# Attention's running state made compact and updated in one step, and work reordered around the two joints of a three-stage kernel

## What is computed

```
for b in range(nb):                                   # attention, 2 batches, 8 heads, 768 tokens, 64 per head
    intra = einsum(qb, kb) * Dmask; intra = einsum(intra, vb)
    inter = einsum('bhid,bhde->bhie', qb * lam_pow, kv_state)
    out[:, :, sl] = intra + inter
    kv_state = lam_block * kv_state + einsum('bhsd,bhse->bhde', kb * rev_pow, vb)
x = out.transpose(0, 2, 1, 3).reshape(1536, 512)
for e in range(4):                                    # mixture of 4 experts, 512 -> 1024 -> 512
    out += p[:, e:e + 1] * (maximum(x @ w1[e], 0) @ w2[e])
a = x @ w1; b = x @ w2                                # gated product, 512 -> 1024
return (((a * b) @ w3) @ w_out)                       # w3 @ w_out is folded into one matrix first
```

## Times and profile before

| | us |
|---|---|
| median of 3 runs (796.08 to 797.36) | 796.5 |
| the profiled execution, its own time | 793.99 |
| its span, first to last instruction | 792.2 |
| PE busy in the span | 776.9 |
| DVE, POOL, ACT busy | 442.4, 439.7, 207.8 |

### The profile page before, as it was taken

How to read it: one execution, slowest core, us unless ns; L and a number is a source line. 1 busy time by engine, 2 the same in 40 slices (tenths; PEclk the granted TensorE clock), 3 DMA queues, 4 the chain that set the end, 5 groups by cost and what they waited for, 6 DMA issues and landing times.

```text
span 792.2 us, 9983 instructions
## 1 busy us (share of the span) xinstructions
PE 776.9 (98%) x3854; PEld 642.5 (81%) x3854; DVE 442.4 (56%) x627; ACT 207.8 (26%) x292; POOL 439.7 (56%) x389
## 2 busy tenths in 40 slices
PE   9999889999999999999999999999998899999998
PEld 7878768888888888888888888888886788888887
DVE  7549874554545545545545455456378653636356
ACT  7423331122222212221222122122234331223110
POOL 8837586557546565665575565656657533342500
PEclk9999999999999999999999999999999999999999
DMA  9977111010210110210100111101000200100004
GB/s 336 342 260 235 61 73 53 2 53 27 67 53 1 54 55 0 86 40 22 53 23 32 53 41 54 54 0 54 27 26 1 72 11 25 54 28 0 1 1 159
DMA packets 26590, 51.29 MB, mean 65 GB/s; under 512 B 3112, under 2 KB 9008, under 8 KB 26544
## 3 DMA queue, kind: packets, MB, share of 16 engines
q1 hardware_dynamic: 26384, 50.64, 18.9%
q10 hardware_dynamic: 160, 0.02, 0.0%
HBM read 45.38 MB, written 5.28 MB: 64 GB/s over the span
## 4 chain that ended last, share of the span: by engine, by line
PE 92%; DVE 4%; POOL 2%; issue 1%; ACT 0%; ACTq 0%; DVEq 0%
PE banks L1303 41%; PE banks L1276 27%; PE banks L1286 15%; PE banks L1189 5%; PE banks L1201 1%; DVE probs L869 1%; PE banks L1233 1%; PE banks L1225 1%; DVE qs L879 1%; POOL xs_l L524 1%; POOL hl L524 1%; PE banks L1249 0%; DVE t L908 0%; PE banks L1241 0%; POOL w_l L524 0%
## 5 line engine op out<-in xcount | busy, mean ns | idle before, releaser
L1010 DVE TENSOR_TENSOR acc<-banks,acc 128x512 f32<-128x512 f32 x215 | 147.1, 690 | 148.3 <-PE banks L1303 135.8
L524 POOL TENSOR_TENSOR hl<-ring,hh 128x512 fp32r<-128x512 f32 x96 | 138.3, 1454 | 162.1 <-ACT hh L630 162.1
L630 ACT ACTIVATE hh<-ring 128x512 fp32r<-128x512 f32 x120 | 75.7, 632 | 404.6 <-DVE ring L987 345.8
L524 POOL TENSOR_TENSOR w_l<-up_raw,w_h 128x1024 fp32r<-128x1024 f32 x43 | 103.4, 2406 | 90.8 <-ACT w_h L630 90.8
L1303 PE MATMUL banks<-hh,d_h 128*128 128x512 f32 x384 | 149.5, 389 | 2.0 <-POOL hl L524 2.0
L1303 PE MATMUL banks<-hh,d_l 128*128 128x512 f32 x384 | 149.4, 389 | 0.0
L1303 PE MATMUL banks<-hl,d_h 128*128 128x512 f32 x384 | 149.4, 389 | 0.0
L1276 PE MATMUL banks<-xs_h,w_h 128*128 128x512 f32 x336 | 131.2, 390 | 5.5 <-DVE u L968 4.7
L1276 PE MATMUL banks<-xs_h,w_l 128*128 128x512 f32 x336 | 130.8, 389 | 0.0
L1276 PE MATMUL banks<-xs_l,w_h 128*128 128x512 f32 x336 | 130.7, 389 | 0.0
L1303 PEld LDWEIGHTS banks<-hh,d_h 128*128 128x128 f32 x384 | 72.1, 188 | 17.3 <-issue 2.4
(11 more groups left out here) (139 smaller groups left out, 992.7 us busy)
## 6 DMA issues: line engine op xcount, KB each, us to landing
dn_raw<-in_moe_w SPq DMA_DIRECT2D x16, 512.0 KB, 3.3
up_raw<-in_moe_w SPq DMA_DIRECT2D x14, 512.0 KB, 3.3
w_raw<-in_w3T SPq DMA_DIRECT2D x16, 256.0 KB, 6.4
up_raw<-in_w SPq DMA_DIRECT2D x8, 512.0 KB, 3.3
pb<-route_scratch SPq DMA_DIRECT2D x12, 256.0 KB, 3.3
out<-acc SPq DMA_DIRECT2D x11, 256.0 KB, 2.0
wo_raw<-in_w_out SPq DMA_DIRECT2D x8, 256.0 KB, 5.3
chunk_w<-in_kT SPq DMA_DIRECT2D x8, 256.0 KB, 5.3
```

The lines of the kernel that those rows point to most:

```text
L524: return tt(dst, whole, high.bitcast(F32), ALU.subtract)
L630: return nc.scalar.activation(dst, src, ACT.Copy)
L1010: tt(cols, group_bank(g), cols, ALU.add).then_inc(acc_done, 1)
```

## The change

**State.** `state` becomes [128, HP, 64]: head 2p in rows 0 to 63 and head 2p+1 in rows 64 to 127 of column block p. `s_dec`, its POOL instruction, the semaphore `state_decayed` with its waits on DVE and SP, and the memset of `state` on POOL with its wait on DVE go. `keep_state` is one copy of 128x256 in a batch's first chunk, and otherwise four instructions that multiply by the decay and add the new part. `from_state` issues eight matmuls with 64 rows and 64 columns of the array each, where four took all of it. The two row halves of the array both write the one bank `out_bank(i)`, into different partitions.

**First joint and first runs.** The low part of `T2` is made half by POOL (k = 0) and half by DVE (k = 1, new semaphore `t2_lo`). POOL makes the third hidden low part of run 0 before `d_low(0)`, not after. In run 1 PE does P1 and P6 ahead of groups 0 to 3 of run 0, not between them; DVE takes `sum_u2(1)` ahead of those groups' evacuations.

**Second joint.** The sums for run NQ+1 move from DVE to POOL, right behind `a_low(NQ + 1)`; ACT's `s_high(NQ + 1)` moves from behind factor "P2" to between the copies of `B11` and `B21`; DVE's `weight_sums_low(NQ + 1)` moves from behind `sum_c22` to ahead of `t3_low(1)`.

```diff
-        state = place(c_at, "state", [P, HP, 2, D])
+        state = place(c_at, "state", [P, HP, D])
...
-                if 1 <= n < NT - 1:
-                    pool.wait_ge(state_ready, updates(i - 1))
-                    tt(s_dec..., state..., q_pow[:, :, P - 1:P].to_broadcast([P, HP, 2 * D]), ALU.mult)
...
-            t_low(0, T2, T2_AT)
+            pool.wait_ge(t_hi, 2)
+            low(xs_l[:, T2, 0, :], T2_AT[:, 0, :], xs_h[:, T2, 0, :]).then_inc(tp_lo, 1)
...
                 hidden_low(OUTS * w + 1)
-                d_low(w)
-                for k in range(2, OUTS):
+                if w > 0:
+                    d_low(w)
+                hidden_low(OUTS * w + 2)
+                if w == 0:
+                    d_low(w)
+                for k in range(3, OUTS):
                     hidden_low(OUTS * w + k)
...
             a_low(NQ + 1)
+            sums(NQ + 1)
...
             b_high(B11, slice(0, KH), slice(0, CW), grouped(NQ - 1, 0) - KH)
+            s_high(NQ + 1)
             b_high(B21, slice(KH, KT), slice(0, CW), grouped(NQ - 1, 0))
...
+                new = kv_bank[:, 0:HP * D].rearrange("p (a e) -> p a e", a=HP)
+                if n == 0:
+                    nc.vector.tensor_copy(state[:, :, :], new).then_inc(state_ready, 1)
+                    return
+                for a in range(HP):
+                    last = nc.vector.scalar_tensor_tensor(out=state[:, a, :], in0=state[:, a, :],
+                                                          scalar=q_pow[:, a, P - 1:P], in1=new[:, a, :],
+                                                          op0=ALU.mult, op1=ALU.add)
...
+            dve.wait_ge(t_hi, 2)
+            sub(xs_l[:, T2, 1, :], acc[:, 1, 0:CW], xs_h[:, T2, 1, :]).then_inc(t2_lo, 1)
...
+            weight_sums_low(NQ + 1)
             t3_low(1)
...
                         b22_low()
-                        weight_sums(w + 1)
...
-                for p in range(HP):
-                    last = mm(out_bank(i)[:, p * P:(p + 1) * P], state[:, p, :, :], qs[:, i % 2, p, :],
+                for h in range(H):
+                    p, r = divmod(h, 2)
+                    rows = slice(r * D, (r + 1) * D)
+                    last = mm(out_bank(i)[rows, p * P:(p + 1) * P], state[rows, p, :], qs[rows, i % 2, p, :],
                               start=False, stop=True, skip_group_check=True)
...
+                if w == 1:
+                    p1(w)
+                    p6(w)
+                    groups(w - 1, (0, 1, 2, 3))
```

More of the change, by code:

```diff
@@ L165, in attention_moe_projection @@
         probs = place(c_at, "probs", [P, H, P])
-        s_dec = place(c_at, "s_dec", [P, HP, 2, D])
         decay = place(c_at, "decay", [P, H, P])
@@ L241, in attention_moe_projection @@
         blank_ready = sem("blank_ready")
-        zeros_ready, state_zero, pow_ready, route_ready = (
-            sem("zeros_ready"), sem("state_zero"), sem("pow_ready"), sem("route_ready"))
+        zeros_ready, pow_ready, route_ready = sem("zeros_ready"), sem("pow_ready"), sem("route_ready")
         pool_chain, dve_chain = sem("pool_chain"), sem("dve_chain")
@@ L477, in _ @@
             nc.gpsimd.memset(zeros[:, :], 0.0).then_inc(zeros_ready, 1)
-            nc.gpsimd.memset(state[:, :, :, :], 0.0).then_inc(state_zero, 1)
             A = stack[:, 0, :]
@@ L535, in _ @@
                        ALU.mult).then_inc(k_decayed, 1)
-                if 1 <= n < NT - 1:
-                    pool.wait_ge(state_ready, updates(i - 1))
-                    tt(s_dec[:, :, :, :].rearrange("p a r e -> p a (r e)"),
-                       state[:, :, :, :].rearrange("p a r e -> p a (r e)"),
-                       q_pow[:, :, P - 1:P].to_broadcast([P, HP, 2 * D]), ALU.mult).then_inc(state_decayed, 1)
                 if 1 <= i <= ST:
@@ L786, in _ @@
                         factor(0, "P2", bank_x)
-                        s_high(w + 1)
                         d_high(hidden_of(w))
@@ L1002, in add_group @@
                 if g == 0:
-                    dve.wait_ge(tp_lo, 6)
+                    dve.wait_ge(tp_lo, 5)
+                    dve.wait_ge(t2_lo, 1)
                 if g == GR * NQ:
-                    dve.wait_ge(tp_lo, 12)
+                    dve.wait_ge(tp_lo, 11)
                 if Q in (0, NQ):
@@ L1054, in _ @@
                 else:
-                    add_groups(w - 1, (0, 1, 2, 3))
+                    if w > 1:
+                        add_groups(w - 1, (0, 1, 2, 3))
                     sum_u2(w)
+                    if w == 1:
+                        add_groups(w - 1, (0, 1, 2, 3))
                     add_groups(w - 1, (4, 5))
@@ L1343, in p6 @@
                 if w in (0, NQ):
-                    pe.wait_ge(tp_lo, 4 if w == 0 else 8)
+                    pe.wait_ge(tp_lo, 3 if w == 0 else 7)
+                if w == 0:
+                    pe.wait_ge(t2_lo, 1)
                 product(bank_y, w % 2, S2, T2, True)
@@ L1382, in p5 @@
                 if w == NQ:
-                    pe.wait_ge(tp_lo, 10)
+                    pe.wait_ge(tp_lo, 9)
                 product(bank_z, w % 2, S1, T1, True)
@@ L1389, in p4 @@
                 if w in (0, NQ):
-                    pe.wait_ge(tp_lo, 6 if w == 0 else 12)
+                    pe.wait_ge(tp_lo, 5 if w == 0 else 11)
                 product(bank_y, w % 2, A22, T4, False)
@@ L1411, in _ @@
             for w in range(1, NQ):
[L1412 to L1415, removed]
+                if w == 1:
+                    p1(w)
+                    p6(w)
+                    groups(w - 1, (0, 1, 2, 3))
+                else:
+                    groups(w - 1, (0, 1))
+                    p1(w)
+                    groups(w - 1, (2, 3))
+                    p6(w)
                 groups(w - 1, (4, 5))
```

12 lines of the change are left out of this document (3 added, 9 removed).

## The result

| | before | after |
|---|---|---|
| median of the runs taken together | 796.93 us (4 runs, 796.08 to 798.42) | 788.31 us (4 runs, 788.09 to 788.55) |
| ratio after to before, 95% interval | | 0.989 (0.9873 to 0.9907) |
| profiled execution | 793.99 us, clock 1.0 | 788.36 us, span 786.6, clock 0.998 |

The forecast of 789.2 is 0.9 above the median, and the time lies in the range. But the two ways of measuring disagree: medians fall by 8.6 us, profiled executions by 5.63. The forecast's sum was 7.3. Which of its terms is right can't be read from the total, so I go place by place.

The account below looks back on a forecast made before the run. PE was taken as the bound, with DVE also full in attention and PE waiting at two joints. Terms 3.2 + 2.6 + 1.5 = 7.3 us off 793.99 gave 786.7, or 789.2 against the 796.5 median; range 787.0 to 793.5.

Parts of the forecast that it names:

- Term 1: Attention: cheaper from_state passes on PE and shorter state updates on DVE save 3.2 us.
- 16 passes in 0.88 for 8 in 1.12: Attention, PE: from_state as 16 quarter-tile passes takes 0.88 us, saving 0.24 per chunk.
- Four updates in 0.64: Attention, DVE: four overlapping 128x64 state updates take 0.64 us; the mask behind starts at 0.56 for 0.88, 0.32 saved.
- Chunks 7 and 8 at 4.0 us, DVE's pace: Attention, batch 2: DVE sets the pace, 4.3 us a chunk before, 4.0 after the change.
- Rival D: More than forecast: scaling at 0.7 to 1.05, p4 starts at 612; terms 1 and 3 rise by 0.7 and 1; 787.5; chance 0.12.
- Term 2: First joint: PE's waits of 0.50 and 1.97 us go, with two restarts of 0.08: 2.6 us.
- Term 3: Second joint: DVE loses four sums, POOL's T4 low part ends at 613.1, p4 starts there for 614.60: 1.5 us.
- rival A: Port by turns, POOL and DVE exclude each other: term 3 is 0.3, first joint costs 0.5; 790.9 us; chance 0.27.
- 7.7 alone and 2.0 for 3.3 us of DVE work: Second joint: POOL's six low parts take 9.7 us, 7.7 alone plus 2.0 beside DVE; 2.3 for 3.7 after the change.
- a sign that it would be wrong: Second joint: a PE wait that grows to 3 us in sum; listed among what would show the forecast wrong.
- B: Attention, DVE: short updates not short, four at 0.42 us make 1.68 for 0.85; 796.1 us; chance 0.07.
- C: Attention, PE: row halves go in turn, from_state takes 2.26 us; 801.4 us, slower; chance 0.04.

Follow-up runs that it names:

- experiment 6: Changed kernel with attention's state as before (block-diagonal, decayed on POOL, two adds on DVE), only its products on 64x64 tiles: 791.3 us.
- experiment 7: Changed kernel with the compact state decayed on POOL again and added on DVE in one 128x256 instruction: 787.56 us, ratio 0.989.
- Experiment 9: Kernel of experiment 7 with the last run's weight-sum low parts moved behind sum_c21(NQ) on DVE: 786.71 us, ratio 0.9881.
- experiments 11 and 12: 11: changed kernel with 8 unused matmuls on PE ahead of P6(NQ)'s wait, 788.33 us; 12: changed kernel again, no edit, 788.18 us.
- experiment 4: Kernel before with the second joint's order alone (last run's weight sums on POOL, s_high copy and weight_sums_low moved): 794.27 us, ratio 0.9975.
- experiment 5: Kernel before with 13 unused matmuls on PE ahead of p4(NQ)'s wait at the second joint: 794.43 us, ratio 0.9979.
- experiments 9 to 12: Adds 10: experiment 9's kernel, T1's low part on DVE, DVE's T3 low part held for T2's, B22's behind sum_u3: 786.97 us.

## Why the prediction was right, and where it was not

The range held, and of the three terms the first two came out near their sizes. That the total came within 0.9 us is luck: the third term was 1.3 us too high, and some 2.3 us that the sum had no term for more than made up for it.

- **Term 1, 3.2 forecast, 2.85 measured** (2.88 in the kernel with that part alone). The sum held, the steps did not. *16 passes in 0.88 for 8 in 1.12*: 1.02 for 1.06. Both old prices are lengths, of a piece of the chain or as modelled; from start to start the same trace has 1.06 and, for L1225's 16 passes, 0.97:

```profile
59.54 1.13 PE L1233 MATMUL banks<-qs,state 128*128 128x128 f32 x8
60.60 0.69 PE L1241 MATMUL banks<-chunk_w,k_dec 128*64 128x64 f32 x16
61.12 1.05 PE L1225 MATMUL banks<-probs,chunk_w 128*64 128x128 f32 x16
62.09 1.16 PE L1201 MATMUL banks<-chunk_w 64*128 64x128 f32 x16
```

  So chunks 2 to 5 gained 0.1 each (0.04 of it the passes; the rest, that DVE's row of 3.72 us no longer sets the pace, as it still does in experiment 6), and to the start of chunk 5's `from_state` it was 0.83, where the forecast's steps make 0.43 + 4 x 0.24 = 1.39. *Four updates in 0.64*: 0.85, about 0.19 apart, not 0.14. *Chunks 7 and 8 at 4.0 us, DVE's pace*: 3.60, PE's pace (table above), because the scaling fell to 0.68 and `t` to 0.41. The forecast kept both at their stretched length though it had itself noted that `s_dec` leaves POOL; "which only gives it room" is the sentence that failed. And the one-step update, which the forecast booked as a gain of 0.32 a chunk, takes 0.85 where the add alone on the same compact state takes 0.41 (experiment 7). Rival D had named the shorter scaling, with 0.12.
- **Term 2, 2.6 forecast, 2.85 measured**, and 2.5 by the runs of the kernel with that part alone. Both waits went, P1 and P6 covered `d_l` and the hidden low parts as forecast. `d_l` took 2.85 us, not 2.41, covered too.
- **Term 3, 1.5 forecast, 0.17 measured.** That is rival A's case at the second joint, for which it had 0.3. The failed step is the one from "7.7 alone and 2.0 for 3.3 us of DVE work" to 2.3 for 3.7 us: POOL's row took 11.1 us, 3.4 more than alone. The 3.3 us counted the second sum (611.65 to 613.02), which ends behind the row (612.74), and the forecast left out `t4_sum`, which now lies beside the row's start:

```profile
602.01 1.22 DVE L929 TENSOR_TENSOR acc<-acc 128x1024 f32<-128x1024 f32 x1
```

```profile
597.25 1.22 DVE L923 TENSOR_TENSOR acc<-acc 128x1024 f32<-128x1024 f32 x1
```

  That is before and after, with the row from 603.07 and from 597.66. DVE's row came later, as the sum for `T1` took 2.25 us for 1.23 (591.37 and 597.14), a delay that the forecast had as covered. Counted so, by estimate from these rows, POOL paid 2.0 us for 3.0 of DVE's work before and 3.4 for 4.5 now: what came on top was paid nearly in full. Experiment 9 took 1.22 out and shortened the row by 0.9. The Trainium skill, SBUF — State Buffer, section SBUF: two separate sides, calls the shared port an exclusive lock. The trace agrees for what came on top (1.4 us for 1.5); the row as a whole stays 1.0 or 1.1 us below the sum of both engines' work. P6's wait is 1.97, not 1.4. It does hide in the wait for T4, as forecast; experiments 11 and 12 show this. At the full clock PE's two waits sum to 3.18 us (experiment 4), which the forecast had named as a sign that it would be wrong, and for this term it was.
- **What the sum had no term for.** The forecast took the difference between the profiled execution and the median (2.5 us) as an offset that stays. It was the second joint's clock, and it left with the 3.13 us wait: 2.4 us of experiment 4 and 1.9 of experiment 5. Without it the sum would have been 5.87, 790.6; with 1.3 too much in term 3 and about 2.3 too little here, the total came out within 0.9.
- **Rivals.** B (updates at 0.42 each) and C (row halves in turn) did not occur: 0.85 for four, 1.02 for 16. The rule quoted for C, on row tiles in one PSUM bank, did not bind here; these halves write different partitions. A's cost of 0.5 at the first joint did not appear.
- **The 1.5 us ahead of `sum_u3(NQ+1)`** stayed, at 1.53 or 1.54 in the changed kernel and in experiments 9 to 12. That it comes from a hidden low part beside POOL's `w_l` was argued from the rows and not tried.

## What to carry to other kernels

The state made compact with its decay left on POOL gained 3.84 us in attention; taking the decay off POOL on top of that gained nothing and gave 0.97 back. Much of the gain came on DVE's other operations, which stand up to 1.0 us longer beside a two-operand instruction on POOL, and an engine that is rid of one instruction does its next one earlier, where it can meet something else. So look at what comes to stand beside what, not only at what goes. Price work that is added to such a neighbourhood nearly in full, at the joints too, and ask of each instruction in it whether it is due there. And before taking one profiled execution as the base of a sum, look at how its clock and time stand in the runs: a median 2.5 us above it was a cost with a place, behind PE's one long wait, and a term like the others.

## What the runs showed of the hardware

- A wait of 3.13 us on PE left the clock at 1.0 in one execution of the same kernel and at half in another (0.43 us between matmuls for 0.227, some 5.7 us long, 2.75 us lost). With 13 unused matmuls in the wait ten of twelve runs kept it. After a wait of 1.97 both occurred too (0.50 at 603 to 606 in one, 1.00 in the other). How long it stays down differs between executions, and why is open.
- From start to start, 16 passes on 64x64 tiles in four quadrants took 1.02 us, and 8 passes on 128x128 tiles with zeros in half of the weights 1.06 ahead of `update` and 0.88 in the last chunk (93.59 to 94.47): the same work at about the same price. 16 passes on 128x64 tiles side by side (L1225) took 0.97.
- A DVE update of 128x64 from PSUM takes 276 ns, four in a row 0.85 us; one of 128x256 takes 0.41. The split by column block costs twice the whole.
